# Delta rule: Gram operands in 4 KB rows, late norms moved behind the first inverse, VectorE takes four rounds of each inverse

## The reference

```python
k_n = k / (norm(k) + 1e-6)
for t in range(S):                       # one state of 48 x 48 per batch and head
    y[t] = q[t] @ state
    v_old = k_n[t] @ state
    state = state + beta[t] * outer(k_n[t], v[t] - v_old)
x = y as (B*S, 384)
h = x @ w_in;  g = P(h) / (Q(h) + 1e-6);  x = g @ w_out          # first layer
h = x @ w_in;  g = h * tanh(softplus(h)); out = g @ w_out        # second layer
```

## Time and profile before

| | |
|---|---|
| median of 3 runs | 1186.69 us (1183.19 to 1191.79) |
| profiled execution | 1183.53 us, span 1181.7 us |
| delta rule | up to 333.2 us of the span |
| busy | TensorE 90%, VectorE 80%, ScalarE 65%, GpSimd 15% |
| granted clock, mean | 0.961 |

### The profile page before, as it was taken

The page is one execution under the profiler, slowest core; times in us unless marked ns, Lnnn a source line. Parts: engine busy times, 40 slices in busy tenths (PEclk is TensorE's granted clock), DMA queues, the critical chain, the costliest instruction groups (busy, mean ns, idle before and its releaser), DMA issues.

```text
span 1181.7 us, 22178 instructions
## 1 busy us (share of the span) xinstructions
PE 1062.4 (90%) x9290; PEld 866.7 (73%) x9335; DVE 949.8 (80%) x1045; ACT 768.2 (65%) x1040; POOL 171.5 (15%) x328
## 2 busy tenths in 40 slices
PE   2187988999978899999999999889999999999997
PEld 2176867877766677777777777668888888888885
DVE  4774656466559999999999999999888788888785
ACT  2333554475557677786777778777676767667664
POOL 2068786764000000000000000000000000000000
PEclk9986889798989999999999999999999999999999
DMA  9615466343221010010100002131010101010000
GB/s 211 168 53 126 130 129 149 97 128 92 94 94 54 1 54 1 0 54 0 54 0 28 26 1 107 54 97 64 1 55 0 53 0 53 1 54 1 19 9 27
DMA packets 28569, 69.02 MB, mean 58 GB/s; under 512 B 3680, under 2 KB 11360, under 8 KB 28000
## 3 DMA queue, kind: packets, MB, share of 16 engines
q1 hardware_dynamic: 28224, 66.98, 20.3%
q10 hardware_dynamic: 256, 0.79, 0.3%
HBM read 53.60 MB, written 14.16 MB: 57 GB/s over the span
## 4 chain that ended last, share of the span: by engine, by line
DVE 34%; PE 33%; issue 3%; ACT 2%; DVEq 0%; ACTq 0%
PE o_ps L819 6%; PE o_ps L821 5%; PE o_ps L820 5%; PE h_ps L821 5%; PE h_ps L819 5%; PE h_ps L820 5%; DVE val L1004 5%; DVE val L1023 5%; DVE val L1036 5%; DVE g_lo L1042 5%; DVE den L996 5%; DVE den L1031 4%; DVE pa L1002 4%; PE h_ps L863 0%; ACT den L883 0%
## 5 line engine op out<-in xcount | busy, mean ns | idle before, releaser
L892 ACT ACTIVATE g_hi<-val 128x1024 fp32r<-128x1024 f32 x96 | 102.0, 1062 | 102.4 <-DVE val L1036 96.4
L819 PE MATMUL o_ps<-g_hi,w_hi_late 128*128 128x512 f32 x288 | 116.4, 404 | 22.1 <-DVE g_lo L1042 22.1
L1036 DVE SCALAR_TENSOR_TENSOR val<-den,val 128x1024 f32<-128x1024 f32 x96 | 117.7, 1226 | 10.7 <-DVE den L1031 0.5
L819 PE MATMUL o_ps<-g_hi,w_hi_early 128*128 128x512 f32 x288 | 114.0, 396 | 12.8 <-ACT stage L929 9.2
L1042 DVE SCALAR_TENSOR_TENSOR g_lo<-val,g_hi 128x1024 fp32r<-128x1024 f32 x96 | 117.6, 1225 | 1.6 <-ACT g_hi L892 1.5
L819 PE MATMUL h_ps<-x_hi,w_hi_early 128*128 128x512 f32 x288 | 113.0, 392 | 2.0 <-DVE val L1004 2.0
L819 PE MATMUL h_ps<-x_hi,w_hi_late 128*128 128x512 f32 x288 | 112.5, 391 | 1.6 <-DVE w_lo_late L87 1.6
L820 PE MATMUL o_ps<-g_lo,w_hi_late 128*128 128x512 f32 x288 | 113.8, 395 | 0.0
L821 PE MATMUL o_ps<-g_hi,w_lo_late 128*128 128x512 f32 x288 | 113.5, 394 | 0.0
L821 PE MATMUL o_ps<-g_hi,w_lo_early 128*128 128x512 f32 x288 | 112.8, 392 | 0.0
L820 PE MATMUL o_ps<-g_lo,w_hi_early 128*128 128x512 f32 x288 | 112.8, 392 | 0.0
(11 more groups left out here) (112 smaller groups left out, 2345.8 us busy)
## 6 DMA issues: line engine op xcount, KB each, us to landing
w_raw<-w SPq DMA_DIRECT2D x16, 768.0 KB, 5.4
kv_run<-kv_n SPq DMA_DIRECT2D x24, 384.0 KB, 4.8
x_raw<-x_dram SPq DMA_DIRECT2D x12, 768.0 KB, 5.6
kq_run<-kq_t SPq DMA_DIRECT2D x44, 192.0 KB, 3.6
kq_gram<-kq_t SPq DMA_DIRECT2D x10, 768.0 KB, 13.6
x_dram<-stage SPq DMA_DIRECT2D x24, 192.0 KB, 4.4
x_dram<-stage SPq DMA_DIRECT2D x6, 768.0 KB, 4.3
out<-stage SPq DMA_DIRECT2D x5, 768.0 KB, 4.1
```

The source lines that it names most:

```text
L819: nc.tensor.matmul(dst, hi, rhs_hi, start=first, stop=False)
L892: act_fn(g_hi[:, n % 2], val[:, n % 2], ACT.Copy, scale=-1.0).then_inc(g_hi_ready, 1)
L1036: dve_stt(val[:, e], den[:, e], 2.0, val[:, e], ALU.subtract, ALU.mult).then_inc(g_ready, 1)
```

## The change

- BURST goes from 13 to 12; new are EARLY = 20 and HEAD = 4.
- kq_gram is loaded by chunk: eight transfers of 4 KB rows per tile in place of two of 16 KB rows, each chunk with a semaphore of its own; chunks 0 and 1 behind c = 1, chunks 2 and 3 behind c = 2. `gram_fill` waits for its two chunks.
- At the start SP issues k_norm of tile 0, then kq of chunks 2 and 3, then beta and the masks; it waits for tile 0's fills before it goes on to kv. ScalarE loads the table with the square root first.
- `sums(2)` moves from ahead of tile 0's inverse to behind the first step; `roots(2)`, `root_inverse(2)`, `weights(2)` and the fills for tile 2 move by one step.
- From tile 2 on the buffer of the inverse is blanked by a load of the unit matrix, and VectorE does the first four of 31 rounds (`first_rounds`, behind step 5, in tile 0 behind step 6); GpSimd does the other 27.
- Both halves of `turn_x` stand behind step 6 (step 7 in tile 0).
- TensorE does 20 `keep_warm` at the very start, and a burst of 12 ahead of the first solve of tile 1, behind the end of tile 1's inverse.

```diff
-        def substitute(eng, tt, j, own, step, done):
-            for r in range(C - 1, 0, -1):
+        def substitute(eng, tt, j, own, step, done, first, last):
+            for r in range(first, last, -1):
...
-            def load_gram(j):
+            def load_gram(j, c):
                 if j >= 2:
-                    sp.wait_ge(gram_done, 4 * j)
+                    sp.wait_ge(gram_done, 4 * (j - 1) + 2 * (c // 2) + 2)
+                n = 2 * G2 * V * B * C
                 for r in range(HALVES):
-                    sp.dma_start(kq_gram[rows(r)].rearrange("p c a s t -> p (c a s t)"),
-                                 kq_t[j, r]).then_inc(kq_gram_loaded, 16)
+                    sp.dma_start(kq_gram[rows(r), c].rearrange("p a s t -> p (a s t)"),
+                                 kq_t[j, r][:, c * n:(c + 1) * n]).then_inc(kq_gram_loaded[c], 16)
...
+            def blank(j):
+                sp.wait_ge(x_ready, TURNS * (j - 1))
+                sp.dma_start(inv[:, j % 2].rearrange("p i k -> p (i k)"),
+                             consts[:, C + B:C + B + C * C]).then_inc(eye_loaded, 16)
...
             load_norm(0)
+            for c in range(2, CT):
+                load_kq(sp, 0, c)
             sp.dma_start(beta[:], beta_n.rearrange("t p n -> p t n")).then_inc(beta_loaded, 16)
...
-            load_gram(1)
+            for c in range(CT):
+                load_gram(1, c)
+            sp.wait_ge(gram_done, 4)
...
+                    if c == 0 and tau + 2 < T:
+                        blank(tau + 2)
+                    if c in (1, 2) and tau + 3 < T:
+                        for c2 in range(2 * c - 2, 2 * c):
+                            load_gram(tau + 3, c2)
...
             for j in range(1, T):
+                pool.wait_ge(n_turned_ready, TURNS * (j + 1))
+                first, done = C - 1, 0
                 if j >= 2:
-                    blank(j)
-                pool.wait_ge(n_turned_ready, TURNS * (j + 1))
-                substitute(pool, nc.gpsimd.tensor_tensor, j, 0, inv_step, STEPS * (j - 1))
+                    pool.wait_ge(dve_step, STEPS + 2 * HEAD * (j - 1))
+                    first, done = C - 1 - HEAD, STEPS + (STEPS - 2 * HEAD) * (j - 2)
+                substitute(pool, nc.gpsimd.tensor_tensor, j, 0, inv_step, done, first, 0)
...
+            pe.wait_ge(zeroed, 1)
+            keep_warm(EARLY)
...
+                    fill = s - (1 if tau == 0 else 0)
+                    gram = tau + 2 < T and 0 <= fill < 4
                     if (tau, s) == (0, 0):
                         keep_warm(BURST)
+                    elif (tau, s) == (1, 0):
+                        pe.wait_ge(gram_used, 4 * (tau + 2))
+                        pe.wait_ge(inv_ready, 1)
+                        by_event()
+                        keep_warm(BURST)
+                    elif gram:
+                        pe.wait_ge(gram_used, 4 * (tau + 2) + fill)
+                        keep_warm(WARM)
+                    solve(tau, c, g)
+                    if (tau, s) == (0, 0):
+                        pe.wait_ge(gram_used, 8)
...
+            def first_rounds(j):
+                dve.wait_ge(eye_loaded, 16 * (j - 1))
+                dve.wait_ge(n_turned_ready, TURNS * (j + 1))
+                substitute(dve, dve_tt, j, 1, dve_step, STEPS + 2 * HEAD * (j - 2), C - 1, C - 1 - HEAD)
...
             turn_n(0, half_k, C)
-            sums(2, 0, CG)
             dve.wait_ge(inv_blank, 2)
...
                     if (tau, s) == (0, 0):
-                        root_inverse(2)
...
+                        sums(2, 0, CG)
...
-                    if s == 5 and tau + 1 < T:
-                        turn_x(tau + 1, 0, half_k)
-                    if s == 6 and tau + 1 < T:
-                        turn_x(tau + 1, half_k, C)
+                    if fill == 5 and tau + 2 < T:
+                        first_rounds(tau + 2)
...
+                    if fill == 6 and tau + 1 < T:
+                        turn_x(tau + 1, 0, half_k)
+                        turn_x(tau + 1, half_k, C)
```

More of the change, by code:

```diff
@@ L25 @@
 TURNS = 2
+HEAD = 4
 BANK = 512
-BURST = 13
+BURST = 12
+EARLY = 20
 WARM = 2
@@ L156, in delta_rule @@
         masks_loaded, beta_loaded = sem("masks_loaded"), sem("beta_loaded")
-        kq_gram_loaded = sem("kq_gram_loaded")
+        kq_gram_loaded = [sem(f"kq_gram_loaded{c}") for c in range(CT)]
         k_norm_loaded = [sem(f"k_norm_loaded{i}") for i in range(RING)]
@@ L266, in _ @@
             sp.dma_start(blk_mask[:], consts[:, C:C + B]).then_inc(masks_loaded, 16)
-            for c in range(2, CT):
-                load_kq(sp, 0, c)
             load_norm(1)
-            load_gram(1)
+            for c in range(CT):
+                load_gram(1, c)
+            sp.wait_ge(gram_done, 4)
             for c in range(2):
@@ L276, in _ @@
                 load_kv(0, c)
-            load_gram(2)
+            for c in range(CT):
+                load_gram(2, c)
             for i in range(2):
@@ L335, in gram_fill @@
                         pe.wait_ge(kq_loaded[2 * cp + c2], 32)
-                if j and f == 0:
-                    pe.wait_ge(kq_gram_loaded, 32 * j)
+                if j and r == 0:
+                    for c2 in range(2):
+                        pe.wait_ge(kq_gram_loaded[2 * cp + c2], 32 * j)
                 if j >= 2:
@@ L441, in _ @@
                     if not gram:
-                        if tau + 2 < T and s == 4:
+                        if tau + 2 < T and fill == 4:
                             pe.wait_ge(gram_used, 4 * (tau + 2) + 4)
@@ L506, in _ @@
                 act.sem_inc(hand.y_stored[cp], 32)
+            nc.scalar.preload_act_table_set("sqrt_and_others")
             for c in range(2):
@@ L513, in _ @@
             squares(2)
-            roots(2)
             squares(3)
@@ L529, in _ @@
                         spread_x(tau + 1, 0)
+                    if (tau, c) == (0, 0):
+                        roots(2)
                     copy_y(tau, c, 1)
```

43 lines of the change are left out of this document (18 added, 25 removed).

## The result

| | runs | median us | ratio to before, 95% interval | profiled execution, span us | granted clock |
|---|---|---|---|---|---|
| before | 4 | 1185.09 | | 1183.53, 1181.7 | 0.961 |
| after | 4 | 1170.85 | 0.9879 [0.9834, 0.9924] | 1168.60, 1167.0 | 0.950 |
| after, again | 13 | 1176.47 | 0.9912 [0.9867, 0.9957] | 1194.01, 1192.4 | 0.921 |

The kernel is faster by 1.2%, and by 0.9% beside the later experiments. Each ratio leaves out the runs that lie more than 1.5% above the fastest run of their kernel, and is taken to the runs of before made beside them. The forecast was 1170 us. Whether its parts were right is another matter, and the trace answers it part by part.

The account below looks back on a forecast made before the run. The chain of waits bounds it; only the delta rule before 333.2 us changes, slowed by TensorE's stops near Gram loads. Terms -8.1 - 25.8 + 5.0 + 2.0 + 4.8 + 5.5 = -16.6 give 1166.9 us profiled, median 1170; forecast's range 1160 to 1180, overall 1153 to 1193.

Parts of the forecast that it names:

- Gram loads, -25.8: Tiles 0 to 2: 4 KB rows end TensorE's stops for late instructions, 30.6 us less 1.6 left per tile.
- The front, -8.1: Ahead of tile 0's inverse: without tile 2's sums in VectorE's queue it starts at 27.08 instead of 35.16 us.
- next late is nothing: Start of tile 0's inverse: once the sums leave, nothing else delays it beyond 27.08 us, so 8.1 us are gained.
- covered until 20.2: At the start: beta may come 1 to 2 us later, hidden by the wait for tile 1's sums; otherwise 2 us.
- Rounds, +5.0: Step 5 (6 in tile 0): VectorE's four rounds exceed its 0.89 us idle by 1.24 us, four times.
- turns, +4.8: Tiles 1 to 4: two turns behind one step stick out by 1.4 us instead of about 0.2, +1.2 each.
- Tile 0, +1.24, +2.0 and +5.5: Tile 0: rounds on the path, their stretching beside GpSimd, and turns, copies and solve at its end (9.7 against 4.2 us).
- For dips of the clock behind the new waits I add nothing: Delta rule steps: half clock behind new waits costed at 0, because tile 3, the measure, already contains one dip.
- The first (no stops, -31): Rival, chance 0.12: no stops remain and no half clock is inherited, about -31 us, 1156.
- The second (packet size gives 1.5 us a stop): Rival, chance 0.20: smaller Gram packets save only 1.5 us per stop, sum +4.6, 1191 us.
- The third: Rival, chance 0.13: waits from VectorE's rounds and turns take the clock to half, 27 us back, +10, 1197 us.
- The fourth: Rival, chance 0.05: GpSimd's inverse becomes the bound in tile 1, +4 on the forecast, 1174 us.

Follow-up runs that it names:

- b_double: Kernel before with Gram loads in 4 KB rows, one burst, those of tiles 3 to 5 issued twice, the copy unread: 1172.16 us, 0.9871 of before.
- b_chunks: Kernel before with only the Gram loads changed, to 4 KB rows by chunk in two bursts: 1163.99 us, 0.9816 of before.
- c_two: Kernel before with 4 KB Gram loads in two bursts and tile 2's sums behind tile 0's inverse, nothing else: 1164.54 us, 0.9846 of before.
- a_pool: Changed kernel with all 31 rounds of the inverses of tiles 1 to 5 on GpSimd: 1177.00 us, 0.9938 of before.
- a_back: Changed kernel with all rounds on GpSimd, turns singly behind steps 5 and 6, no burst ahead of tile 1: 1178.67 us, 0.9924 of before.
- a_turn0: Changed kernel with tile 0's pair of turns one step earlier, behind step 6: 1171.76 us, 0.9919 of before.
- c_weights: c_two with the next residual behind the norms and weights in VectorE's first step of each tile: 1162.53 us, 0.9751 of before.
- a_solve: Changed kernel with TensorE's wait for scale_gram and its keep_warm behind the solve: 1180.63 us, 0.9949 of before.
- b_once: Kernel before with Gram loads in 4 KB rows, all eight of a tile issued behind c = 1: 1174.97 us, 0.9899 of before.
- a_whole: Changed kernel with the Gram loads put back to two of 16 KB rows per tile: 1201.83 us, 1.0119 of before.

## Why the prediction was right, and where it was not

**The total** came within a microsecond of 1170 in the first four runs and 6 us above it in the thirteen later ones; the change of the profile came within two (-14.7 against -16.6). Part of that agreement is luck. By the remainders only 5.6 us of the 14.7 are the code's own; the other 9.0 are 20.5 us less at half clock, in this execution. (At 0.37 in place of 0.44 it is 7.1 and 7.6.) The second profile of after has 112.6 us at half clock, 37.5 more than before. Over all runs the mean is 69 us against 83 in before. I had put nothing in the range for what the clock does from run to run. And the terms missed in opposite directions: the loads and the front gave less than I had put, the rounds and turns cost less.

**Gram loads, -25.8: the mechanism right, the size near.** Alone they give -20.3 us of median (1184.25 to 1163.99), taken out of the change they cost 25 to 31. In the profiles it is -21.5 and -26.7, roughly half stops and half clock behind them. Of these 4.6 and 3.4 us come ahead of the first u_blk, where the forecast had none of it, so that 17 and 22 us are left for the tiles. The mechanism, an instruction block that comes late, is what the packets on q8 show: TensorE goes on 1.24 to 1.65 us behind the landing of one. b_double shows that in the steps the size of the rows matters and their amount does not. The 1.6 us per tile that I left in, 4.8 in all, had no ground: the wait at 262.1 is no stop for instructions but the wait for the residual, in all 14 profiles, and in the steps of after the longest stop inside a group is 0.92 us.

What is not shown is why one stop lasts 4 us. A 16 KB packet was estimated at 1.8 us of its engine (the trace has 1.65 in the median), and taking turns packet by packet (the Trainium skill, DMA: Bandwidth & Descriptors, "Queues, rings and completion order") would make an instruction block wait for about one, if what the trace lists as a packet is one for the engine too, which no run shows. Of the 4.51 us at 100.3 in before, 1.6 pass until the instruction packet starts, about one such turn, 1.6 while it moves and 1.3 from its landing to the next multiplication. But at 16.8 it is 2.9 us until the packet starts, and when a block was asked for no view shows; whether an instruction block waits more than once on its way was not tried.

**The front, -8.1: the step "next late is nothing" failed.** It gave -6.2 in the first profile and -7.9 in the second. The prediction's own sign of being wrong, that the inverse's start has found another wait, came true. Next late is TensorE's last fill of tile 0, for which VectorE waits 2.19 us. The forecast took 27.08 for the time at which nothing else is late, but 1.35 us of waiting for this fill were in it already, behind a stop of 6.17 us. In after the first fill starts 3.7 us later, because its kq operands land later, and the stop of 5.00 us follows. Beta "covered until 20.2" held: it comes at 15.35 after a wait of 4.25 us, and VectorE afterwards still waits for ScalarE and for TensorE. That the late kq operands come from the new order of the loads or from the early multiplications was not separated. And I missed that the Gram loads in 4 KB rows shorten the wait for ScalarE by themselves (4.6 us in b_chunks), so that the two edits share this gain.

**Rounds, +5.0, and turns, +4.8: each step as foretold, the sum not.** A step with rounds is 1.2 us longer. But the pair of turns in the next one costs 0.3 in tiles 1 to 3 (4.45 against 4.2) rather than 1.2, and a tile's last step is 0.3, 0.7 and 0.8 shorter than in c_two. In tiles 1 to 4 the remainders of after and c_two differ by 0.8 us in all, where the forecast had 8.5. The failed step is the one that let each late VectorE operation stick out by its full length beyond the idle 0.89: what is late in one step is in part made up in the next. a_pool and tile 4 show it from the other side, for where no rounds stand ahead, the pair of turns does cost 1.0 (5.2 us in a_pool, 6.85 against 5.83 in tile 4). Two edits that took rounds and turns off again (a_pool, a_back) found no gain in the medians.

**Tile 0, +1.24, +2.0 and +5.5: the sum right, the parts not all.** Its remainder is 9.1 us above c_two's; the forecast had 8.7. The end is 9.15 us as foretold (9.7). The stretch of the rounds beside GpSimd did not occur: GpSimd was through with tile 1's inverse at 96.4, and the rounds began at 99.10 and took 2.1 us. In tiles 1 to 3 GpSimd waits for the rounds, so the two never work beside each other there, and the price taken from the earlier trace rows was not tested. Of the 9.1, a_pool takes off 1.7 and a_back 3.8 more; the other 3.6 go with the wait of TensorE for `scale_gram` in the second step, 3.17 us against 1.57 in c_two, and what else was not separated. That the burst "keeps the clock up for tile 1" failed. It ends 2.67 us before x_blk is there, and the first step of tile 1 has half clock for most or all of it in the five profiles with the turns at the end of tile 0 (7.9 to 8.4 us); where the turns stand earlier (a_turn0, a_back, c_two) it has full clock and takes 6.1 to 6.5, with the burst or without.

**"For dips of the clock behind the new waits I add nothing": the weakest step.** The norms of tile 2 "just stall the second step in place of the first" is where it went: 3.17 us of wait at 69.77, and half clock for the two steps behind it, 8.5 and 8.8 us. The same wait in tile 3, 1.74 us, has 8.1 and 8.0 behind it. c_weights, with this wait shortened, has the shortest steps there, but not less half clock over its runs. And a_solve took it off in after and gained nothing.

**The rivals.** The first (no stops, -31) was not reached, but its loads were: b_chunks has no stop over 1.1 us in its steps. The second (packet size gives 1.5 us a stop) is refuted by b_chunks. The third had its mechanism, waits for VectorE with half clock behind them, and a wrong place: behind the second step, not behind rounds and turns. That taking VectorE's work off brings no less half clock (75 and 82 us over the runs of a_pool and a_back, 69 in after) speaks against its cause. The fourth did not occur: GpSimd's last operation of tile 2's inverse ends at 134.8, and it is turned at 147.49.

**What stays open.** What sets the time at half clock. In single profiles a_pool, a_back and b_once have 80 to 90 us where after and b_chunks have about 50, but over all runs a_pool and after do not differ by more than their errors; b_chunks (56 ± 5) against b_once (76 ± 6), and a_solve (86 ± 6) against a_turn0 (59 ± 3), seem to, and no cause was tried. And 7 us of remainder between a_back and c_two, 2.5 of them ahead of the first u_blk and 3.6 in tile 0, were not traced to one edit among the early multiplications, the new waits of SP, the later fills of tile 0 and the loads of the unit matrix.

## What to carry to other kernels

When an engine stops in the middle of a group with no semaphore to wait for, look for a packet of instructions that lands just before it goes on, and at what the DMA engines carry just then: loads in rows of 16 KB were worth 20 us to cut into rows of 4 KB, though no one waited for their data. Before a wait is laid to instructions, look whether a semaphore is behind it. Judge an edit by the part of its time that the clock does not explain, from more than one profile, and by medians of many runs (each run's span and mean clock are enough for that); and try the parts of a change one by one, for here one part alone (0.9816) is better than the whole (0.988 to 0.991). The version to keep is c_two or c_weights, which the runs do not tell apart: 4 KB rows and late sums, with nothing of the division of the inverse.

## What the runs showed of the hardware

- TensorE's stops inside a group end 1.24 to 1.65 us behind the landing of a 16 KB packet on q8, in 46 cases of 46 over 14 profiles.
- Time at half clock costs 0.44 of itself by one pair of profiles and 0.37 by 176 runs, and it varies between runs of one kernel: 54.6 and 112.6 us in two profiles of after, 1165.11 to 1194.01 us over 13 runs.
- A wait of TensorE of 1.7 to 3.2 us had half clock for one or two steps behind it more often than not, but the 3.17 us at 109.28 had only one such step behind it (8.1, then 5.1 us), and in b_double 78.5 us at half clock came with no stop over 1.6 us but the waits for `scale_gram`.
- 4 KB rows moved 315 GB/s over 14 us in b_double; a load in 16 KB rows came with 247 GB/s over 18 us in a_whole, and 192 over 18 us in before with 147 at the plateau. A data packet of 16 KB took 1.65 us in the median, one of 4 KB 0.21 (before).
- A shown clock of 1.00 ahead of the record's first entry says nothing: in c_two multiplications of 0.61 to 0.63 us stand beside it, the length that they have at half clock (0.38 at full).
